# VectorE rounds the high part of g in layer 2, in place of ScalarE

## What is computed

```python
kv = einsum('bhsd,bhse->bhde', k, v)            # attention without a softmax
out = einsum('bhsd,bhde->bhse', q, kv)
x = out / sqrt(mean(out * out, -1) + 1e-6) * g_norm      # 4 x 8 heads x 576 x 64
x = x.transpose(0, 2, 1, 3).reshape(2304, 512)
h = x @ w_in1; x = (h * sigmoid(1.702 * h)) @ w_out1     # layer 1, 512 -> 2048 -> 512
h = x @ w_in2; out = softplus(h) @ w_out2                # layer 2: max(h,0) + log1p(exp(-|h|))
```

## Time and profile before

| | |
|---|---|
| device time, median of 3 runs | 975.18 us (974.70 to 975.87) |
| the profiled execution | 979.29 us, span 977.5 us |
| TensorE busy | 848.5 us (87%), weight loads 756.4 us |
| VectorE busy | 590.0 us (60%) |
| ScalarE busy | 428.1 us (44%) |
| GpSimd busy | 227.0 us (23%) |
| transfers | 139.26 MB, 142 GB/s over the span |
| granted TensorE clock, mean | 0.955 of full |

### The profile page before, as it was taken

How to read it: one execution, slowest core, us unless ns; L and a number is a source line. 1 busy time by engine, 2 the same in 40 slices (tenths; PEclk the granted TensorE clock), 3 DMA queues, 4 the chain that set the end, 5 groups by cost and what they waited for, 6 DMA issues and landing times.

```text
span 977.5 us, 12329 instructions
## 1 busy us (share of the span) xinstructions
PE 848.5 (87%) x4584; PEld 756.4 (77%) x4584; DVE 590.0 (60%) x1024; ACT 428.1 (44%) x815; POOL 227.0 (23%) x261
## 2 busy tenths in 40 slices
PE   6867898959989879989897989977998987899897
PEld 6756888958889868889887878766887876778785
DVE  4654656665655575664576666666666666666663
ACT  4642232233122123122137565655656556665654
POOL 1598666251232141352421100000000000000000
PEclk9997999979999989999899999998999998999998
DMA  9933537232452642554452242231524222432401
GB/s 309 335 126 118 211 145 291 97 151 97 170 228 98 235 163 98 186 231 164 175 191 98 76 150 77 87 119 37 199 75 144 83 76 76 151 139 76 150 2 64
DMA packets 25674, 139.26 MB, mean 142 GB/s; under 512 B 2448, under 2 KB 8208, under 8 KB 18448
## 3 DMA queue, kind: packets, MB, share of 16 engines
q1 hardware_dynamic: 25040, 138.16, 38.6%
q10 hardware_dynamic: 576, 0.33, 0.1%
HBM read 104.40 MB, written 34.08 MB: 142 GB/s over the span
## 4 chain that ended last, share of the span: by engine, by line
PE 43%; DVE 18%; ACT 16%; DMA 8%; issue 8%; POOL 6%; SPq 0%; ACTq 0%; DVEq 0%
PE ps L549 22%; PE ps L594 10%; PE ps L588 7%; DMA w_in_f<-w_in 5%; DVE gs_f L880 5%; PE ps L591 4%; ACT ex L705 4%; ACT fix L707 3%; ACT ex L703 3%; ACT gs L713 3%; DVE gs_f L888 3%; DVE gs L891 2%; DMA kv_in_sb<-k_v 2%; DVE xs L847 2%; DVE xs_f L839 2%
## 5 line engine op out<-in xcount | busy, mean ns | idle before, releaser
L549 PE MATMUL ps<-xs,w_in 128*128 128x384 f32 x2016 | 424.7, 351 | 86.7 <-DVE gs_f L880 73.9
L549 PEld LDWEIGHTS ps<-xs,w_in 128*128 128x128 f32 x2016 | 366.3, 197 | 120.6 <-issue 80.4
L594 PE MATMUL ps<-w_out,gs 128*128 128x512 f32 x864 | 230.5, 405 | 23.3 <-DVE gs L913 23.3
L880 DVE TENSOR_TENSOR gs_f<-ps,gs_f 128x384 f32<-128x384 f32 x240 | 132.9, 554 | 174.2 <-PE ps L549 170.4
L588 PE MATMUL ps<-gs,w_out 128*128 128x512 f32 x576 | 211.2, 399 | 3.1 <-POOL w_out L418 3.1
L594 PEld LDWEIGHTS ps<-w_out,gs 128*128 128x128 f32 x864 | 164.7, 194 | 56.6 <-issue 29.5
L591 PE MATMUL ps<-gs,w_out 128*128 128x256 f32 x576 | 163.6, 284 | 0.0
L588 PEld LDWEIGHTS ps<-gs,w_out 128*128 128x128 f32 x576 | 110.9, 193 | 22.1 <-POOL w_out L418 3.4
L591 PEld LDWEIGHTS ps<-gs,w_out 128*128 128x128 f32 x576 | 111.5, 194 | 0.0
L697 ACT ACTIVATE lg<-gs_f 128x384 f32<-128x384 f32 x72 | 37.1, 523 | 159.2 <-DVE gs_f L880 159.2
L913 DVE TENSOR_TENSOR gs<-gs_f,gs 128x384 fp32r<-128x384 f32 x96 | 54.1, 564 | 84.0 <-ACT gs L713 81.6
(11 more groups left out here) (58 smaller groups left out, 593.3 us busy)
## 6 DMA issues: line engine op xcount, KB each, us to landing
w_in<-w_kept SPq DMA_DIRECT2D x40, 1792.0 KB, 7.3
w_kept<-w_in SPq DMA_DIRECT2D x16, 1792.0 KB, 8.2
kv_in_sb<-k_v SPq DMA_DIRECT2D x16, 512.0 KB, 10.7
w_in_f<-w_in SPq DMA_DIRECT2D x16, 512.0 KB, 8.1
w_out_f<-w_out SPq DMA_DIRECT2D x16, 512.0 KB, 8.8
q_sb<-q_t SPq DMA_DIRECT2D x16, 288.0 KB, 11.1
out<-xy SPq DMA_DIRECT2D x18, 256.0 KB, 7.7
tail_sb<-k_v SPq DMA_DIRECT2D x3, 256.0 KB, 12.8
```

The lines of the kernel that those rows point to most:

```text
L549: mm = nc.tensor.matmul(ps[:, bank, 0:HALF], w[:, wp, W_OF[k], cols], xs[:, k, xp, t], start=(new and t == 0 and (wp, xp) == (HI, HI)), st ...
L594: mm = nc.tensor.matmul(ps[:, ACC_BANK + j, 0:DM], g[:, j * P:(j + 1) * P], w, start=new, stop=done)
L880: nc.vector.tensor_tensor(to, bank, other, ALU.add).then_inc(added, 1)
```

## The change

`round_g` and its calls go from ScalarE's queue. `low_g` on VectorE gets the cast: it waits on `soft_made`, which VectorE itself counts up, casts, waits for the cast by `g_hi_late`, and subtracts. The numbers the semaphores are waited for are the old ones. Nothing is changed on TensorE, GpSimd and SP, nor in layer 1.

```diff
--- before.py
+++ after.py
@@ -708,10 +708,6 @@
                     act.wait_ge(one_more, i1 + 1)
                     nc.scalar.activation(lg[:, i % 2], fix[:, i % 2], ACT.Ln).then_inc(log_made, 1)
 
-            def round_g(m, tile):
-                act.wait_ge(soft_made, TILES * (m - PHASE1) + tile + 1)
-                nc.scalar.copy(g_high(m, tile), hid(m, tile)).then_inc(g_hi_late, 1)
-
             def round_w_in(d):
                 b = split_buffer(d)
                 act.wait_ge(w_summed, 4 * d + 4)
@@ -754,8 +750,6 @@
             for m in range(ALL):
                 ci, p = m // STEPS, m % STEPS
                 first_product(m)
-                if m > PHASE1:
-                    round_g(m - 1, C12)
                 if p == STEPS - 1 and m < ALL - 1:
                     round_x(ci + 1, B11)
                 hidden(m, C11)
@@ -770,8 +764,6 @@
                 if p == 0 and ci > 0:
                     round_x(ci, B22)
                     round_x(ci, T1)
-                if m >= PHASE1:
-                    round_g(m, C11)
                 if p == 0 and ci > 0:
                     copy_sums(ci - 1, 0, 3)
                 hidden(m, C21)
@@ -780,16 +772,11 @@
                 hidden(m, C22)
                 if p == 0 and ci > 0:
                     copy_sums(ci - 1, 3, ACC_BANKS)
-                if m >= PHASE1:
-                    round_g(m, C21)
                 if m == 0:
                     round_w_out(m)
                 hidden(m, C12)
                 if m == PHASE1 - 1:
                     nc.scalar.preload_act_table_set("natural_log_exp_and_others")
-                if m >= PHASE1:
-                    round_g(m, C22)
-            round_g(ALL - 1, C12)
             copy_sums(2 * CHUNKS - 1, 0, ACC_BANKS)
 
 
@@ -909,7 +896,10 @@
                 nc.vector.tensor_tensor(low, low, ex[:, i % 2], ALU.subtract).then_inc(soft_made, 1)
 
             def low_g(m, tile):
-                dve.wait_ge(g_hi_late, TILES * (m - PHASE1) + tile + 1)
+                i1 = TILES * (m - PHASE1) + tile
+                dve.wait_ge(soft_made, i1 + 1)
+                nc.vector.tensor_copy(g_high(m, tile), hid(m, tile)).then_inc(g_hi_late, 1)
+                dve.wait_ge(g_hi_late, i1 + 1)
                 nc.vector.tensor_tensor(g_low(m, tile), hid(m, tile), g_high(m, tile).bitcast(F32),
                                         ALU.subtract).then_inc(g_split, 1)
```

## The result

The changed kernel takes 927.16 us, median of 4 runs (925.24 to 930.14), beside 975.52 (974.70 to 977.99, 4 runs) for the kernel before on the same chip: a ratio of 0.9503, 95% interval 0.9469 to 0.9537. The forecast was 926, with a range of 919 to 937.

The account below looks back on a forecast made before the run. Chain latency, not a full engine, was taken as the bound. Terms 28.4 + 6.8 + 6.5 + 1.6 (tail) + 5.8 (clock) = 49.1 us off the median 975.18 gave 926, range 919 to 937.

Parts of the forecast that it names:

- What bounds the kernel: Layer 2: no engine is full; a chain's latency decides, with VectorE standing 78.5 us for ScalarE's cast.
- The cast: Layer 2 on VectorE: 0.36 us per cast, as in layer 1; last softplus operation to low part 0.98.
- ScalarE's lost load: ScalarE loses 96 casts of 510 ns, 49 us, worth 0 by themselves because it is not full.
- A steady step: Layer 2: P1's wait goes, 0.05 us of wait remains at the six down products, which start 1.63 earlier.
- The term of 28.4 us: Steady steps of layer 2: 15 pairs of waits at 1.63 us plus 3 single C22 waits at 1.3.
- Late next: Steady step: P2 waiting for ScalarE's copy of P1, P7 for U2, and VectorE's added work, all costed at 0.
- The ends and begins of chunks: Ends (m = 31, 39): 3.4 us each, 6.8 in all; begins (m = 24, 32, 40): 6.5 us in all.
- The term for m = 24: Begin of the chunk at m = 24: an estimated 1.9 us, where GpSimd works beside it; 2.3 at the other begins.
- The clock: Full clock kept in the tail (2.8 us) and at P1 after three chunk begins (1.0 each): 5.8 us.
- The rivals: Clock falls all the same, 932 (0.18); the wait moves, 935 (0.13); nothing changes, 975 (0.02); slower, 995 (0.03).
- The slower rival: C21 and C22 in each step: VectorE's queue pays more for casts than it waited; 20 us, 995; chance 0.03.

Follow-up runs that it names:

- the run with the load put back: Changed kernel with ScalarE keeping 96 casts of the same size at their old queue places, written to a tile nothing reads: 933.52 us.
- the single tiles: Kernel before with only one tile's cast on VectorE: C21 946.90 us, C22 960.56, C11 969.94, C12 972.60.
- GpSimd busy: Changed kernel plus 12 unread GpSimd adds (128 x 256) per step from m = 26: 1000.14 us; kernel before with the same adds: 1001.58 us.
- after: The changed kernel itself, all four casts of layer 2 on VectorE, against the kernel before: 927.16 us, ratio 0.9503.

## Why the prediction was right, point by point

**What bounds the kernel.** A chain's latency, and in it VectorE waiting in line: shown from both sides. With ScalarE's load put back the steady step stays at 15.94; with each cast on VectorE 0.4 us longer, and two of them in the chain, it is 0.8 longer.

**The cast.** 0.36 taken, 0.36 median measured. From L909 to the low part 0.98 forecast, 0.98 to 0.99 measured.

**ScalarE's lost load.** Counted at 0. That holds in a steady step; over the whole the run with the load put back gained some 5 us less, of which the profile places 0.5 to 0.8 at the begin of each chunk.

**A steady step.** Forecast 17.57 less 1.63, or about 15.94, with both waits gone; measured 15.94 with both gone. Its split, P1's wait by C21 and the down products' by C22, is what the single tiles show: 0.9 and 0.7 of it. The term of 28.4 us stands.

**Late next.** Nothing in a steady step: P2 and P7 wait for nobody. At a chunk's begin P2 waits 0.40 us for the copy of P1 where 0.5 was forecast.

**The ends and begins of chunks.** Their terms came out near: in the ledger 17.1 and 14.6 us for the two whole chunks, where 16.2 each was forecast. The end of a chunk was right: the three down products at 644.53 and 781.90 both start 4.35 us earlier, counted from P1 of m = 31 and 39, where the forecast has 3.4 and 1.0 of the steady step. What differs is the clock behind them. In the second chunk it stays low longer, and from those products to P1 of m = 41 only 1.1 us were gained, where the first chunk gained 3.0 and the forecast has 2.3. So the sum of the two came out near because one lay above and one below. The term for m = 24 was a little too large: 1.9 forecast, 1.4 measured. What was wrong in its working is the share of the tiles: the wait before P1 was laid to the waits of C11 and C21 together, and C21 alone took it from 2.77 to 1.47.

**The clock.** Counted as kept, 5.8 us, and it was kept in all four places: P1 of m = 25, 33 and 41 and the tail. The Trainium skill, "TensorE: Matmul & The Clock Gate", What's actually happening, calls the low clock the default and ties the high one to recent activity; the tail agrees, 8.44 us after a wait of 1.06 beside 11.24 after 2.81. That waits of at most 1.6 keep the clock at the begin of a chunk holds in every run: 24 waits of 0.74 to 1.58 before P1 of m = 25, 33 or 41 were all followed by full clock. But that the longer waits cost it was less certain than the working had it, which knew only that 1.38 us of nothing costs no clock and 2.75 does. In the runs a wait of 1.84 was followed by low clock in m = 33 and not in m = 41 (the cast made twice), and one of 2.05 in 10 of 14 (GpSimd busy). With C12 alone on VectorE the waits of 2.77 (m = 25) and 2.81 (the tail, 36 products in 8.44) were followed by full clock, though they were as long as before. So part of the 5.8 us may be luck of the one profiled execution: that every execution of before pays all of it is not shown.

**The sum.** 926 forecast, 927.16 measured; the chip's own runs of before stood 0.3 above those of the forecast, so the gain was 48.4 where 49.2 was forecast. That the two agree to 1 us is in part luck: the clock at the chunk ends alone moved single terms by 1 us and more. The rivals are out: no new wait in a steady step, no lower clock where it was counted as kept, no bound by VectorE. The slower rival has a real mechanism all the same. Its point was a cast of 1.1 us, with nothing else changed; beside GpSimd it decides at 0.76 already, because the operations around the cast lengthen too and take VectorE's spare time.

## What to carry to other kernels

When an engine that works in order stands waiting for a short helper operation that another engine queues behind its own long work, give the operation to the waiting engine, even if it is the busier one: here 96 x 0.36 us more work on VectorE bought 48 us. Read the gain from the two waits of TensorE and the margin between them, not from the waits of VectorE (78.5 us here) nor from ScalarE's freed time (49 us, worth nothing in a steady step and some 5 us in all). And look at who shares memory with the receiving engine in that stretch: with GpSimd at work the same move was worth nothing.

## What the runs showed of the hardware that was not expected

- GpSimd at work lengthens VectorE's operations with two inputs in SBUF by more than the cast: 0.56 to 0.98 us for 128 x 384 (L906, L913), up to 1.09 for L899 and L902, and 0.36 to 0.76 for the cast. The add that reads PSUM (L877) stays at 0.54, and ScalarE's cast at 0.51.
- One long wait of TensorE can cost more than two short ones of the same sum: 2.05 was followed by low clock in 10 of 14 steps (1.3 us each), 0.81 and 1.37 in none of 14.
- The length of a wait doesn't settle the clock behind it: 1.84 was followed by low clock in one place and by full clock in another of the same run, and so was 2.26 in after (641.15 and 778.52). Waits of 2.77 and 2.81 (C12 alone) and 3.27 (C11 alone, m = 41: twelve matmuls in 2.32) were followed by full clock.
